# Retention ahead of a mixture of experts: chunk loads issued against landings, weights split into high and low halves in later turns

## What is computed

```python
scores = (q @ k.T) / sqrt(64)                     # 2 x 8 heads, 576 x 576, head size 64
ret = (scores * gamma_h ** (i - j) * (i >= j)) @ v
x = ret as rows of 1152 tokens x 512
p = domain_probs / (domain_probs.sum(-1) + 1e-9)
x = sum_e p[:, e] * (relu(x @ w1[e]) @ w2[e])     # 4 experts, 512 -> 1024 -> 512
h = x @ w_in                                      # 512 -> 2048
out = (h * tanh(softplus(h))) @ w_out             # 2048 -> 512
```

## Time and profile before

| what | value |
|---|---|
| median of 3 runs | 621.39 us (620.98 to 622.14) |
| the profiled execution, its own time | 619.39 us |
| its span, first to last instruction | 617.3 us |
| PE (matmul) busy | 604.9 us, 98% |
| DVE, ACT, POOL busy | 265.1, 234.8, 278.5 us |
| mean granted TensorE clock | 0.997 |
| DMA in the first two fortieths of the span (31 us) | nine tenths busy or more, 345 and 340 GB/s |

### The profile page before, as it was taken

One profiled execution on the slowest core, in us unless ns is written; L12 is line 12 of the kernel. 1 busy time (PEld: TensorE's weight loads), 2 busy tenths in 40 slices (PEclk: granted clock), 3 DMA queues, 4 the chain that ended last, 5 costly groups with the idle time before them and its releaser, 6 DMA issues.

```text
span 617.3 us, 9709 instructions
## 1 busy us (share of the span) xinstructions
PE 604.9 (98%) x3952; PEld 546.4 (89%) x3952; DVE 265.1 (43%) x365; ACT 234.8 (38%) x434; POOL 278.5 (45%) x230
## 2 busy tenths in 40 slices
PE   7799999999999999999999999999999999999997
PEld 5788999999899999999999999989989999989996
DVE  5477654323254433154434154535545432334334
ACT  2466244322233321323332223435455454334431
POOL 2668645534435535335554435532446543443300
PEclk9899999999999999999999999999999999999999
DMA  9963222322112332012331112321112232201002
GB/s 345 340 225 103 72 66 65 109 72 64 35 34 69 107 100 69 34 35 69 102 102 54 50 35 69 103 68 52 52 35 65 67 101 75 69 0 52 2 0 103
DMA packets 24923, 50.47 MB, mean 82 GB/s; under 512 B 2864, under 2 KB 2992, under 8 KB 24880
## 3 DMA queue, kind: packets, MB, share of 16 engines
q1 hardware_dynamic: 24736, 49.84, 25.2%
q10 hardware_dynamic: 144, 0.02, 0.0%
HBM read 47.49 MB, written 2.36 MB: 81 GB/s over the span
## 4 chain that ended last, share of the span: by engine, by line
PE 95%; DMA 2%; issue 1%; DVE 1%; SPq 1%; ACT 1%
PE bank L527 31%; PE bank L529 31%; PE bank L528 31%; DMA w_raw<-in_weights 2%; PE bank L651 1%; PE bank L459 1%; PE bank L489 1%; PE bank L493 1%; SPq L423 0%; DVE acc_sb L945 0%; DVE acc_sb L949 0%; PE bank L464 0%; SPq L420 0%; ACT st L728 0%; ACT xa_hi L734 0%
## 5 line engine op out<-in xcount | busy, mean ns | idle before, releaser
L412 POOL TENSOR_TENSOR w_lo<-w_raw,w_hi 128x512 fp32r<-128x512 f32 x96 | 134.4, 1414 | 147.8 <-ACT w_hi L385 144.3
L527 PE MATMUL bank<-w_hi,h_hi 128*128 128x512 f32 x432 | 168.7, 390 | 0.0
L529 PE MATMUL bank<-w_hi,h_lo 128*128 128x512 f32 x432 | 168.4, 390 | 0.0
L528 PE MATMUL bank<-w_lo,h_hi 128*128 128x512 f32 x432 | 168.3, 390 | 0.0
L932 DVE TENSOR_TENSOR h_act<-part,bank 128x384 f32<-128x384 f32 x96 | 52.9, 552 | 170.4 <-PE bank L529 169.9
L407 POOL TENSOR_TENSOR ws<-ws_f,ws 128x1024 fp32r<-128x1024 f32 x24 | 58.4, 2432 | 144.8 <-ACT ws L381 144.8
L529 PEld LDWEIGHTS bank<-w_hi,h_lo 128*128 128x128 f32 x432 | 81.1, 188 | 16.9
L528 PEld LDWEIGHTS bank<-w_lo,h_hi 128*128 128x128 f32 x432 | 81.1, 188 | 12.3
L527 PEld LDWEIGHTS bank<-w_hi,h_hi 128*128 128x128 f32 x432 | 81.0, 188 | 12.1
L764 ACT ACTIVATE part<-bank 128x384 f32<-128x384 f32 x72 | 35.4, 491 | 138.8 <-PE bank L529 138.8
L899 DVE SCALAR_TENSOR_TENSOR h_lo<-h_act,h_hi 128x384 fp32r<-128x384 f32 x64 | 73.3, 1155 | 20.9 <-ACT h_hi L754 20.3
(11 more groups left out here) (98 smaller groups left out, 867.6 us busy)
## 6 DMA issues: line engine op xcount, KB each, us to landing
w_raw<-in_weights SPq DMA_DIRECT2D x144, 256.0 KB, 2.7
loaded<-in_toks SPq DMA_DIRECT2D x9, 512.0 KB, 7.7
loaded<-in_feats SPq DMA_DIRECT2D x8, 512.0 KB, 7.0
out<-acc_sb SPq DMA_DIRECT2D x6, 256.0 KB, 2.1
out<-acc_sb SPq DMA_DIRECT2D x1, 768.0 KB, 3.5
loaded<-in_first SPq DMA_DIRECT2D x1, 726.0 KB, 4.5
ident<-in_ident SPq DMA_DIRECT2D x1, 64.0 KB, 4.7
p_nat<-in_probs ACTq DMA_DIRECT2D x1, 18.0 KB, 5.3
```

The source lines that it names most:

```text
L412: pool.tensor_tensor(w_lo[layer][:, x], w_raw[:, r % RAW], w_hi[layer][:, x].bitcast(F32), ALU.subtract).then_inc(s_wl, 1)
L527: pe.matmul(out, w[0], x[0], start=first, stop=False, **more)
L528: pe.matmul(out, w[0], x[1], start=False, stop=False, **more)
L529: return pe.matmul(out, w[1], x[0], start=False, stop=last, **more)
```

## The change

Three things. SP's queue: from chunk 4 on each load is issued only when an earlier one has landed (two chunk loads or one and a weight on their way), one weight ahead of each chunk in place of two, and from then on up to weight 13 a load waits for the one three before it. The constant `ident` is loaded after weight 13. `JOBS_IN`: the first weight job stands in turn 2 and not 1, most others a turn later, and the first sum (`s`, 0, 0) at the end of turn 9 and not in turn 7. ACT and POOL: in turn 3 ACT makes the `hi` of the turn's first job ahead of tile 0's; POOL does a turn's jobs ahead of `v_decay` of two chunks on; the first sum's `hi` stands on ACT behind the second `t_hi`.

```diff
--- before.py
+++ after.py
@@ -58,11 +58,11 @@
 
 TILE_AMID = {3: 0}
 TILES_IN = {3: (1,), 4: (2,), 5: (3,), 6: (4,), 7: (5, 6), 8: (7,)}
-JOBS_IN = {1: (("w1", 0, 0),), 2: (("w1", 0, 1), ("w1", 0, 2)), 3: (("w1", 0, 3),), 4: (("w1", 0, 4), ("w1", 0, 5)),
-           5: (("w1", 0, 6),), 6: (("w1", 0, 7), ("w2", 0, 0)), 7: (("w2", 0, 1), ("w2", 0, 2), ("s", 0, 0)),
-           8: (("w2", 0, 3), ("w2", 0, 4)), 9: (("w2", 0, 5),)}
-
-WEIGHTS_IN = (2, 2, 2, 2, 2)
+JOBS_IN = {2: (("w1", 0, 0),), 3: (("w1", 0, 1), ("w1", 0, 2)), 4: (("w1", 0, 3),), 5: (("w1", 0, 4),),
+           6: (("w1", 0, 5), ("w1", 0, 6)), 7: (("w1", 0, 7), ("w2", 0, 0)), 8: (("w2", 0, 1), ("w2", 0, 2)),
+           9: (("w2", 0, 3), ("w2", 0, 4), ("w2", 0, 5), ("s", 0, 0))}
+
+PACED = 14
 ROWS_IN = {4: 5, 5: 6, 6: 7, 7: 8}
 PROBS_IN = 5
 WARM_START, WARM_NEXT = 7, 5
@@ -429,21 +429,45 @@
                 sp.dma_start(w_raw[:, r % RAW], weights_in[2 * UNITS * e + UNITS * layer + u])\
                   .then_inc(s_raw[r % RAW], 16)
 
+            def feats_there(c):
+                sp.wait_ge(s_feats[c % SLOTS], landed(c))
+
+            def toks_there(c):
+                sp.wait_ge(s_toks[c % SLOTS], landed(c))
+
+            def weights_there(r):
+                sp.wait_ge(s_raw[r % RAW], 16 * (r // RAW + 1))
+
             sp.dma_start(loaded[:, lead - CONSTS:lead + 2 * KIND], first_in).then_inc(s_feats[0], 16)
             load_toks(0)
             for c in range(1, SLOTS):
                 load_feats(c)
                 load_toks(c)
-            at = 0
-            for c in range(SLOTS, PLACES):
-                for r in range(at, at + WEIGHTS_IN[c - SLOTS]):
-                    load_weights(r)
-                at += WEIGHTS_IN[c - SLOTS]
+            load_weights(0)
+            feats_there(SLOTS - 1)
+            sp.wait_ge(s_o, 1)
+            load_feats(SLOTS)
+            weights_there(0)
+            load_toks(SLOTS)
+            feats_there(SLOTS)
+            load_weights(1)
+            toks_there(SLOTS)
+            for c in range(SLOTS + 1, PLACES):
+                at = c - SLOTS + 1
+                feats_there(c - 1)
                 sp.wait_ge(s_o, c - SLOTS + 1)
                 load_feats(c)
+                toks_there(c - 1)
+                if c == SLOTS + 1:
+                    weights_there(1)
                 load_toks(c)
-            sp.dma_start(ident[:, :], ident_in).then_inc(s_id, 16)
-            for r in range(at, len(LOADS)):
+                weights_there(at - 1)
+                load_weights(at)
+            for r in range(PLACES - SLOTS + 1, len(LOADS)):
+                if r < PACED:
+                    weights_there(r - 3)
+                if r == PACED:
+                    sp.dma_start(ident[:, :], ident_in).then_inc(s_id, 16)
                 load_weights(r)
             by_rows = out.rearrange("(g p) d -> p g d", p=P)
             sp.wait_ge(s_af, read(EXPERTS - 1, TT - 1))
@@ -790,14 +814,20 @@
                 for job in IN_TURN.get(c - 1, ()):
                     if JOBS[job][0] == "s":
                         job_hi(act, job)
+                ahead = 1 if c in TILE_AMID else 0
+                for job in IN_TURN.get(c, ())[:ahead]:
+                    job_hi(act, job)
                 if c in TILE_AMID:
                     plain_hi(*divmod(TILE_AMID[c], ITEMS))
-                for job in IN_TURN.get(c, ()):
+                for job in IN_TURN.get(c, ())[ahead:]:
                     if JOBS[job][0] != "s":
                         job_hi(act, job)
             for n in range(4):
                 t_hi(0, n)
                 if n == 1:
+                    for job in IN_TURN[PLACES]:
+                        if JOBS[job][0] == "s":
+                            job_hi(act, job)
                     for job in IN_STAGE[1]:
                         job_hi(act, job)
 
@@ -1098,10 +1128,10 @@
             v_decay(0)
             v_decay(1)
             for c in range(TURNS):
+                for job in IN_TURN.get(c, ()):
+                    job_lo(pool, job)
                 if c + 2 < PLACES:
                     v_decay(c + 2)
-                for job in IN_TURN.get(c, ()):
-                    job_lo(pool, job)
             pool.wait_ge(s_tl, 4)
             for s in range(1, ALL_STAGES):
                 for job in IN_STAGE.get(s, ()):
```

## The result

The change makes the kernel slower. The median is 623.23 us (620.3 to 625.05, 21 runs) against 621.18 us (619.46 to 623.09, 21 runs): 2.05 us more, a ratio of 1.0032 with a 95% interval of 1.0020 to 1.0044. I had forecast 619.8 us, faster. The profiled execution took 621.12 us with a span of 619.0 us, 1.7 us over that of before.

A forecast was written before the change was run, and what follows sets the result against it. PE was taken to bound it, with matmuls in 604.9 of 617.3 us and a code-packet gap behind data loads. 1.95 + 1.35 + 0.3 - 2.0 = 1.6 us faster: 621.39 to 619.8 us, range 617.9 to 622.0.

The forecast's parts named there:

- 2.0 us lost: At P6 of stage 2: POOL's late sums and low half make it start at 68.6 us in place of 66.64.
- I cost the pacing itself at nothing: Loads in retention: chunks at most one per 4 us stay ahead of PE's one per about 5.3 us; no cost.
- First gap: PE's code gap at 18.85 us: code packet 1.5 to 2 us earlier, tile 0 at 20.4 for 22.41, 1.95 us won.
- clock: After the gap at 18.85 us, in tile 0: PE works more, no fall to half clock, 1.35 us won.
- small gap: PE's gap before tile 1: goes as PE and the code packet come earlier, 0.3 us won.
- rival D: Pacing too tight: weight 1 or 2 lands late and a tile waits 1 us, 620.8 us; chance 0.05.
- Jobs a turn later: Weight roundings moved later in retention: POOL stays about 3 us ahead of tile 7, costing nothing.
- weight sums last: First weight sum moved behind POOL's other jobs: P6 starts later, 2.0 us lost.
- my bound of 2.9: Worst case for the loss at P6: all sums at 0.95 us and w_lo at 2.0 each give 2.9 us.
- Behind P6: After P6 of stage 2: POOL's work is the same in kind and amount as before, costed at nothing.
- Rival A: Gap and lower clock stay at the start, only 0.2 us won, late sums cost 2.0: 623.2 us; chance 0.12.

The follow-up runs named there:

- Experiment 7: Changed kernel with each weight ahead of its chunk's tokens, two weights a chunk from chunk 6, jobs' table of before from turn 5: 619.32 us, 0.9978 of before.
- Experiment 1: Kernel before with only the first weight sum moved, from turn 7 to the end of turn 9: 620.74 us against 620.79, ratio 0.9997.
- experiment 2: Changed kernel's table of jobs and ACT and POOL queues, with the unpaced loads of the kernel before: 625.86 us, ratio 1.0067 to before.
- experiment 6: Changed kernel with turn 9's three w_lo made for 128 of 512 columns, part of the products left out: 618.41 us, ratio 0.9958 to before.
- 8: Changed kernel with each chunk's weight issued ahead of its tokens, its table of jobs kept: 623.14 us, ratio 1.0029 to before.
- 12: The kernel of Experiment 7 run again, unchanged: 619.17 us, ratio 0.9967 to the kernel before.
- 11: The kernel of Experiment 7 with eight matmuls of zeros ahead of the first scores in place of seven: 619.37 us, ratio 0.9970 to before.

## Why the prediction was wrong

I forecast 1.6 us faster and got 2.05 us slower in the median, 1.73 in the profiled execution. The terms that failed are three: "2.0 us lost" at P6, where 3.45 were lost by the time that P6 starts; "I cost the pacing itself at nothing", where 1.2 us of the start's gain went again in retention; and the clock, which the sum left at full speed behind P6's wait. By its own steps:

*First gap, clock, small gap (1.95 + 1.35 + 0.3).* Right in mechanism, and nearly in size in the profiled execution: 1.7, 1.3 and 0.35, 3.35 us won at tile 1 for 3.6. Tile 0 started at 20.69, released by DVE's xa_lo as I had it, for 20.4; the gap was 0.49; the clock stayed. What was wrong is to take one trace of before for the kernel. Gap and fall come elsewhere in another trace, in the changed kernel's second trace the clock fell in tile 0 all the same, and in a late start pacing wins next to nothing at tile 0. So the term is a mean of several cases, and 3.6 is one of them. That a packet of code waits behind data, which this term rests on, is argued from the traces and not shown.

*"I cost the pacing itself at nothing".* Wrong by 1.2 us in this execution: PE arrived at the end of retention 2.1 us early, not 3.35. I took 4.0 us for a load, one chunk per 4 us, and a PE that needs one per 5.3 us. That need was misread from tiles 0 and 1, which hold the lower clock and a gap; from tile 4 to tile 5 of before it is 4.31 us, so the cover was 0.3 us and not 1.3. The loads of the chunks took 3.7 to 5.9 us, a chunk about 5, and each weight stands behind its chunk's tokens, so that tiles 2 to 4 waited for w_lo, 1.3 us in sum: my rival D, which I had given 0.05. The waits and the loss aren't the same 1.3 us, though. At tile 4 the gain was still 3.4 us, as before has two gaps of its own by then; it was lost between tiles 4 and 5, by a gap of 0.79 us without a releaser and some shorter ones. Experiment 7, without waits for w_lo, has `second(0)` at 52.05, only 0.16 us sooner.

*"Jobs a turn later: nothing."* The later jobs put three w_lo behind retention's last tile in place of one, and only with them does the late sum cost. I did count their time, in the term "weight sums last", so nothing is missing from the sum here; but I named the wrong half of the change. Experiment 1 has the sum's move alone at 0.9997, experiment 2 the table at 3.0 us of wait, and experiment 6 removes most of the three w_lo and with it the wait.

*P6 "2.0 us lost".* This is the largest miss. The chain was right: POOL's four sums, then ACT's queue to part and POOL's low half, nearly level, as I had them. The size was 3.0 us of wait, just over my bound of 2.9. POOL began the three w_lo at 53.50 (55.65 less the 2.1 won, as I had it) and took 5.25 for my 5.43. The mis-sized part is the four sums: 3.3 us predicted from 0.75 each, 5.2 measured. I had stretched w_lo for DVE's company and hardly the sums, which stand in the same company. Given that, ACT's and POOL's 4.2 from the sums to P6 were 4.1. Two pieces of 0.2 us, at P1 and between P1 and P6, I had put under P6's wait, but PE lost them besides it. From `second(0)` to P1 it is 8.38 to 8.40 us in the six traces with P6's wait and 8.15 or 8.16 us in the eight others, experiment 6 among them, so the first piece comes with the three w_lo.

*Behind P6, "I cost it at nothing".* 0.4 us. From P6 of stage 2 to that of stage 3 it is 15.95 us for 15.54. Of the traces without a fall of the clock there, those with the sum in turn 9 have 15.80 to 15.96 us (experiments 1, 6 and 8), those with it in turn 7 have 15.54 (7 and 12), so it goes with the sum's place.

*What P6's wait does to the clock.* Missing. I had weighed the clock at tile 0 and not at the one place where I myself forecast a stop of 2 us. It falls in four of six traces. Against the 15.95 us without a fall the stretch behind P6 takes 17.04, 17.21, 17.21 and 18.36 us, so a fall of 3.4 us costs 1.1 to 1.3 us, the one of 6.8 us costs 2.4, and the mean of the six is about 1 us.

Together: 2.1 won at the end of retention, 3.0 lost at P6, and 0.8 in the products round it (0.2 at P1, 0.2 more by P6, 0.4 by stage 3), 1.7 in the profiled execution. The fall of the clock, which that execution didn't have, comes on top in others. The two profiled executions are among the fastest of their kernels, 1.8 and 2.1 us under the medians, so the terms above are those of one pair; how they add up to 2.05 us in the median, with the bad cases that before has too, the runs don't settle.

*Rival A* gave 623.2 and slower, and the number came out. Its mechanism didn't: the gap was gone and the clock stayed, in the profiled execution. That the number fits is luck.

## What to carry to other kernels

When a table moves work later, count what then stands behind the last piece that PE does by itself, on each helper engine: here one more turn's delay put three subtractions, 5.25 us, behind the last tile, where a product of PE had to wait for what POOL makes after them. Hold loads back only as far as the work fed by them can still be done in its old turn; the version that paces and has the old table from turn 5 on is 0.2 to 0.3% under before. Price the clock at each new place where PE stands, not only at the old one: here falls to 0.50 followed stops of 1.3 to 3.0 us, though not all of them (2.24 and 2.34 us in experiments 12 and 11 had none). And take a second trace of the kernel before ahead of a sum of terms of a microsecond: the spans of its two differ by 4.4 us.

## What the runs showed of the hardware that I had not expected

The start has two kinds. In seven of the 14 traces the clock has risen to 1.00 by 5.1 us, in six others only at 9.7 to 10.7 us, with both kinds for the same program (the kernel before); one is between, at 7.1 us. In a late start the second score group comes about 2 us later (PE idle before it until 13.0 to 13.4 and not 11.2 to 11.7 us).

At the next border of code the time from PE's resuming to the start of the next packet, and the gap that follows, differ with the loads and with the start. With an early start it is 4.0 us with the loads of before (gaps of 2.33 and 2.28 us) and 1.3 to 2.3 us with paced ones (0.49 us or none, six traces). With a late start it is 1.6 and 1.3 us with the loads of before (no gap), although the DMA engines are over nine tenths busy there, and 2.2 to 3.3 us with paced ones (0.37 to 1.51 us, three traces), 3.55 us with three loads added. So the mere share of busy DMA engines doesn't set the delay.

POOL's sum of 128x256 took 0.75 us beside a DVE that waits or reads PSUM, and 0.9 to 1.5 us beside DVE's work in SBUF; DVE's operations of 128x768 there took 1.5 to 2.04 us in place of 0.95.
